# A three-stage kernel on one core: two stages in one block, one wait moved, one subtraction in halves, nine unread products

## The chip, the cores and the metric

The kernel runs on one core of a Trainium2 chip. The metric is the device time of one execution in microseconds (us). Five engines work side by side, each through its own list of instructions, and meet only at semaphores: TensorE (PE; its weight loads are PEld), VectorE (DVE), ScalarE (ACT), GpSimd (POOL) and SyncE (SP), which here only issues transfers. GpSimd also issues the indirect transfers (gather and scatter of rows).

## The reference, cut to what matters

```python
# stage 1, attention with a decaying state: 4 batches, 8 heads, 768 steps, head size 48
S = a * S + k[t] (outer) v[t]                  # a complex, its size bounded by 0.999
y[t] = q[t] @ S.real
# stage 2, on x = y as 3072 rows of 384
h = x @ w_in                                   # 384 -> 2048
x2 = (max(h, 0) + alpha * min(h, 0)) @ w_out   # 2048 -> 384
# stage 3, routed experts
do = x2 @ w_skip > 0                           # the other rows go out as they are
e = argmax(x2 @ w_gate)                        # one of 8 experts; gate = its softmax weight
out[do] = x2 + gate * (max(x2 @ w1[e], 0) @ w2[e])     # 384 -> 1024 -> 384
```

## The kernel before, in words

`build` makes the tensors that all stages share (the eight PSUM banks `mlp_ps`, `out_ps`, `att_ps`, the two halves `arena`, `rows`, `logits`) and calls `phase1` (stages 1 and 2) and then `phase2` (stage 3). Each phase opens a `Block` of its own: a block holds the instruction lists of the five engines, and at its end all engines meet before the next block starts. The SBUF tensors of phase 2 lie where those of phase 1 lay.

**Phase 1** walks over eight halves of 384 rows (`Half`). A half's attention runs beside the two products (`up`, `down`) of the half before. The work of each engine is written out by hand in `step`; the last half has no attention beside it and runs in the loop at the end of each engine's list. For each of 16 tiles `f` of the hidden width, TensorE makes `up(f)` (9 products, L646) into `mlp_ps`; ScalarE makes `bend_h` (L964); VectorE joins both in `join_g` (L1493); ScalarE and VectorE split the result into a high part and a remainder (`high_g` L972, `low_g` L1498); TensorE makes `down(f)` (9 products, L658) into `out_ps[0..2]`. `up(f)` waits for `join_g(f - 2)`, and the last half's list is `up(0)`, `up(1)`, `up(2)`, then `up(f)` and `down(f - 3)` in turn. On VectorE the wait `dve.wait_ge(state_moved, NC * HALVES * 64)` (L1967) stands ahead of the first `join_g` of that last half. `state_moved` counts SyncE's transfers of the attention state to `s_stack` (L382); the last four of them are issued behind the store of the second last half's rows. Nothing reads that last state. At the end ScalarE's `take_x2` (L985, L987) copies, for each of the three banks in turn, nine logits into `logits` and 384 values into `x2` (in `rows`), and SyncE stores `x2` to `out` and to `x2_rows` (L393, L394).

**Phase 2** first works out the routing: VectorE takes the largest logit and the membership (L2309 to L2324) with an index from GpSimd (L2469, L2471); TensorE counts ranks (L2172, L2173); VectorE works out each row's slot (L2337 to L2374) and then the entries of a table (`entries`, L2388), which TensorE sums with 24 products (L2181). Two copies out of the table give the rows to gather and to scatter (`gather_at` L2411, `scatter_at` L2412). GpSimd's `gather` (L2493) fetches 128 rows for a slot. For each slot TensorE turns the rows (L2188), makes the first layer (48 instructions, L2210), turns the next slot's rows, for which it waits until they have been gathered, and makes the second layer (24, L2224). The weights `w2` of an expert are split: ScalarE copies the high part (`split`, L2257), VectorE subtracts it (`split`, L2404, 128 x 3072). VectorE's `split(0)` stands behind the copies of the table, before `keep_x(1)`, which waits for the gathered rows. SyncE loads the weights of experts 1 and 2 at once and those of expert 3 when the first gather has landed (L2145, L2151). The slots of an expert stand in the code as `If` blocks and a loop, so their number is decided by branches.

Of the kernel before, what the change touches and what calls it, by code (L numbers as in the profile page):

```python
# [6 lines left out]
F32 = mybir.dt.float32  # L7
# [12 lines left out]
NC = 3  # L20
# [67 lines left out]
def val(count):  # L88

    return count.value() if isinstance(count, Count) else count  # L90
# [24 lines left out]
def build(nc, qk, v, a, mask_in, w_in, w_pack, alpha, w_skip, w_gate, w1, w2, out, x2_rows):  # L115
    with ExitStack() as ctx:
        def sem(name):
            return ctx.enter_context(nc.semaphore(name))

        def sb(name, shape, dt=F32):  # L120
            return ctx.enter_context(nc.sbuf_tensor(name, shape, dt))

        mlp_ps = [ctx.enter_context(nc.psum_tensor(f"mlp_ps{i}", [P, 512], F32)) for i in range(2)]
        out_ps = [ctx.enter_context(nc.psum_tensor(f"out_ps{i}", [P, 512], F32)) for i in range(3)]
        att_ps = [ctx.enter_context(nc.psum_tensor(f"att_ps{i}", [P, 512], F32)) for i in range(3)]

        ident = sb("ident", [P, P])
        logits = sb("logits", [P, NT, LANES])
        arena = [sb(f"arena{i}", [P, KT * FE]) for i in range(2)]
        rows = sb("rows", [P, NC * DL + DM])  # L130
        x2_stored = sem("x2_stored")
        first_loaded = [sem(f"first_loaded{i}") for i in range(2)]

        phase1(nc, qk, v, a, mask_in, w_in, w_pack, alpha, w_skip, w_gate, w1, w2, out, x2_rows,
               mlp_ps, out_ps, att_ps, ident, logits, arena, rows, x2_stored, first_loaded)
        phase2(nc, w1, w2, out, x2_rows, mlp_ps, out_ps, att_ps, ident, logits, arena, rows, x2_stored, first_loaded)


def phase1(nc, qk, v, a, mask_in, w_in, w_pack, alpha, w_skip, w_gate, w1, w2, out, x2_rows,
           mlp_ps, out_ps, att_ps, ident, logits, arena, rows, x2_stored, first_loaded):  # L140
    with ExitStack() as ctx:
        def sem(name):
            return ctx.enter_context(nc.semaphore(name))

        def sb(name, shape, dt=F32):
            return ctx.enter_context(nc.sbuf_tensor(name, shape, dt))

# [103 lines left out]
        g_lo = sem("g_lo")  # L251
        g_used = sem("g_used")
        x2_taken = sem("x2_taken")

        def att(h, name, c):

# [49 lines left out]
        def of_chunk(x, c):  # L306
            return x[..., c * DM:(c + 1) * DM]

        block = ctx.enter_context(nc.Block())


        @block.sync
# [538 lines left out]
        def _(act):  # L851
# [122 lines left out]
            def pair(n, f):  # L974
                if f < NF:
                    bend_h(n, f)
                if f >= 1:
                    high_g(n, f - 1)

            def take_x2(n):  # L980
                act.wait_ge(g_used, val(n.n * NF + (NF + 4)))
                act.wait_ge(x2_stored, val(n.n * 32 + 1))
                first = (n.n * NC).value()
                for i in range(NC):
                    act.activation(logits[:, bass.ds(first + i, 1), :].rearrange("p a l -> p (a l)"),  # L985
                                   out_ps[i][:, DM:DM + LANES], ACT.Copy)
                    act.activation(x2[:, i, 0:DM], out_ps[i][:, 0:DM], ACT.Copy).then_inc(x2_taken, 1)  # L987
# [304 lines left out]
            last_n = Half(0, HALVES - 1)  # L1292
            for f in range(NF + 1):
                pair(last_n, f)
            take_x2(last_n)


        @block.vector
        def _(dve):
# [664 lines left out]
                step(Half(0, n), True, True)  # L1964
            step(Half(0, HALVES - 1), True, False)
            last_n = Half(0, HALVES - 1)
            dve.wait_ge(state_moved, NC * HALVES * 64)  # L1967
            for f in range(NF + 1):
                pair(last_n, f)


        @block.gpsimd
        def _(pool):
# [6 lines left out]
            for bank in range(3):  # L1980
# [12 lines left out]
def phase2(nc, w1, w2, out, x2_rows, mlp_ps, out_ps, att_ps, ident, logits, arena, rows, x2_stored, first_loaded):  # L1993
    with ExitStack() as ctx:
        def sem(name):
            return ctx.enter_context(nc.semaphore(name))

        def sb(name, shape, dt=F32):
            return ctx.enter_context(nc.sbuf_tensor(name, shape, dt))
# [91 lines left out]
        w2_loaded = [first_loaded[1], *(sem(f"w2_loaded{p}") for p in range(1, BODY))]  # L2091
        w2_hi = sem("w2_hi")
        w2_lo = sem("w2_lo")
        expert_left = sem("expert_left")
        x_gathered = sem("x_gathered")
        x_turned = sem("x_turned")
# [7 lines left out]
        y_stored = sem("y_stored")  # L2104

        NP = NFE // 2
        block = ctx.enter_context(nc.Block())

        def expert(x, e):
            return x[e:e + 1]  # L2110
# [57 lines left out]
        def _(pe):  # L2168
# [5 lines left out]
            for t in range(NT):  # L2174
                if t % GROUP == 0:
# [3 lines left out]
                    else:  # L2179
# [2 lines left out]
                                 entries[t // GROUP][:, t % GROUP, :, :].rearrange("p a s -> p (a s)"),  # L2182
                                 start=(t == 0), stop=(t == NT - 1))
            last.then_inc(table_full, 1)

            def turn_x():
                for kk in range(KT):
# [49 lines left out]

        @block.scalar
        def _(act):
            act.wait_ge(diff_made, 1)  # L2240
            act.activation(expd[:, :, :], diff[:, :, :], ACT.Exp).then_inc(exp_made, 1)
            act.wait_ge(rows_known, 1)
            for t in range(NT - GROUP, NT):
                act.activation(far_off[:, t + GROUP - NT, :], lane[:, :], ACT.Abs, bias=row_of[:, t:t + 1], scale=-1.0).then_inc(distance, 1)
            act.wait_ge(distance, GROUP)
            act.activation(in_row[:, NT - GROUP:NT, :], far_off[:, :, :], ACT.Relu, bias=1.0, scale=-1.0).then_inc(late_rows_made, 1)

            def place_x(s):
                act.wait_ge(x_turned, val(s))
                act.activation(xT[:, :, :].rearrange("p k t -> p (k t)"), att_ps[0][:, 0:DM], ACT.Copy).then_inc(xT_made, 1)  # L2250

            def split(e):
                p = e % BODY
                if e >= BODY:
                    act.wait_ge(expert_left, e - BODY + 1)
                act.wait_ge(w2_loaded[p], e // BODY * 16 + 16)
                act.activation(w2_v[p][0][:, :, :], w2_raw[p][:, :, :], ACT.Copy).then_inc(w2_hi, 1)  # L2257

            count = act.alloc_register("act_slot")
            act.reg_mov(count, 1)  # L2260
            split(0)
            split(1)
            act.wait_ge(slots_known, 1)
            slots_here = slots_of_all(act)
            place_x(1)

            def expert_slots(e):
                n = slots_here[e]

                def split_next():  # L2270
                    if e + 2 < EXPERTS:
                        split(e + 2)

                def slot(is_first=False):
                    s = act.snap(count, min_val=1, max_val=NSLOT - 2)
                    act.wait_ge(b_done, val(s))
                    for g in range(NP):
                        act.wait_ge(h_full, val(s * 4 + (g - 3)))
                        act.activation(hT[:, 0, 2 * g:2 * g + 2, :].rearrange("p f t -> p (f t)"),  # L2279
                                       mlp_ps[g % 2][:, 0:2 * P], ACT.Relu).then_inc(h_hi, 1)  # L2280
                    place_x(s + 1)
                    act.reg_add(count, count, 1)
                    if is_first:
                        split_next()

                with act.If(n > 0):
                    slot(is_first=True)
                    act.nop()
                act.nop()
                if e + 2 < EXPERTS:  # L2290
                    with act.If(n < 1):
                        split_next()
                        act.nop()
# [8 lines left out]
        def _(dve):  # L2302
# [3 lines left out]
            def flat(x):  # L2306
                return x[:, :, :].rearrange("p e t -> p (e t)")

            dve.tensor_scalar(dropped[:, :], skip, 0.0, BIG, ALU.is_le, ALU.mult).then_inc(skips_placed, 1)  # L2309
            dve.tensor_reduce(out=top[:, :], in_=lg, op=ALU.max, axis=AX.X).then_inc(step, 1)  # L2310
            dve.wait_ge(step, 1)
# [89 lines left out]
            def split(e):  # L2401
                p = e % BODY
                dve.wait_ge(w2_hi, e + 1)
                dve.tensor_tensor(w2_v[p][1][:, :, :], w2_raw[p][:, :, :], w2_v[p][0][:, :, :].bitcast(F32), ALU.subtract).then_inc(w2_lo, 1)  # L2404

            dve.wait_ge(table_full, 1)
            dve.tensor_scalar(tab[:, :, 0], att_ps[1][:, 0:NSLOT], FAR, None, ALU.add).then_inc(tab_made, 1)
            dve.tensor_reduce(out=tab[:, :, 1].bitcast(F32), in_=att_ps[1][:, NCOL:3 * NCOL].rearrange("p (a s) -> p s a", a=2)[:, 0:NSLOT, :],
# [1 line left out]
            dve.wait_ge(tab_made, 2)  # L2410
            dve.tensor_copy(gather_at[:, :], tab[:, 0, 0:1]).then_inc(first_at, 1)  # L2411
            dve.tensor_copy(scatter_at[:, :], tab[:, NSLOT - 1, 0:1]).then_inc(first_at, 1)  # L2412
            split(0)
            dve.wait_ge(slots_known, 1)
            slots_here = slots_of_all(dve)
            keep_x(1)
            count = dve.alloc_register("dve_slot")
            dve.reg_mov(count, 1)
            dve.wait_ge(step, val(last_step))
# [43 lines left out]

        @block.gpsimd
        def _(pool):
            pool.sem_inc(b_done, 1)
            pool.sem_inc(y_made, 2)
            pool.sem_inc(h_lo, 4)
# [29 lines left out]
                                        bounds_check=TOKENS - 1, oob_is_err=False).then_inc(y_stored, 16)  # L2498

            pool.wait_ge(pads_made, 1)  # L2500
            pool.wait_ge(first_at, 2)
            gather()
            pool.memset(y[:, :], 0.0).then_inc(pads_made, 1)
            pool.wait_ge(slots_known, 1)
            slots_all = pool.value_load(slots_i[0:1, EXPERTS:EXPERTS + 1], min_val=0, max_val=NSLOT - 2)
# [93 lines left out]
```

## Time and profile before

| | |
|---|---|
| median of 3 timed runs | 857.11 us (855.49 to 857.2) |
| profiled execution, own time | 853.47 us |
| its span in the trace | 851.5 us |
| mean granted TensorE clock | 0.95 |
| busy: PE, PEld, DVE, ACT, POOL | 84%, 81%, 71%, 56%, 6% |

The span is what the trace covers; 1.97 us of the execution's time lie around it. Times in the rows are microseconds from the start of the span. A granted clock of 1.00 is 2.4 GHz and 0.50 is 1.2 GHz. Busy shares are means over stages with different limits, so they do not say what ends a stage; the rows do.

### The profile page before, as it was taken

To read this page: it belongs to the slowest core of one execution; us is meant where nothing else is said; L and a number is where in the kernel's file an instruction comes from. 1 tells how busy PE (TensorE), PEld (TensorE's weight loads), DVE (VectorE), ACT (ScalarE), POOL (GpSimd) and SP (SyncE) were. 2 spreads that over 40 slices of the span, in tenths; PEclk is the share of its full clock that TensorE was granted. 3 is DMA by queue.
4 is the path that set the end of the run, shared out by engine and by line. 5 is a ranking of instruction groups with operands and counts; after the bars stand their busy time and mean duration, and the time that the engine had idled before them with its cause. 6 is when DMAs were issued, how large, how long until landed. Compare 5 with 4: busy or idle time off the path is not lost. (4 is left out here: it accounts for less than half of the span.)

```text
span 851.5 us, 15352 instructions
## 1 busy us (share of the span) xinstructions
PE 718.7 (84%) x5454; PEld 693.5 (81%) x5454; DVE 607.5 (71%) x1250; ACT 478.3 (56%) x937; POOL 54.7 (6%) x56
## 2 busy tenths in 40 slices
PE   1213749999999999999999999999989639899895
PEld 1213749999999999999999999999889539799895
DVE  4986978997997997998899799654333454344442
ACT  8267369479559739937946964843423243233320
POOL 2000000000000000000000000000000122223222
PEclk9998769999999999999999999999989859899999
DMA  5465553345145325515515523442600376914200
GB/s 166 155 204 119 148 153 98 75 121 175 45 122 172 90 60 172 145 48 146 175 34 145 159 74 77 131 121 58 212 26 1 116 278 225 318 39 171 95 27 20
DMA packets 82429, 104.67 MB, mean 123 GB/s; under 512 B 15990, under 2 KB 68384, under 8 KB 82336
## 3 DMA queue, kind: packets, MB, share of 16 engines
q1 hardware_dynamic: 79648, 98.44, 38.9%
q0 software_dynamic: 1792, 3.76, 1.4%
q10 hardware_dynamic: 896, 1.25, 0.6%
q8 instruction: 56, 0.92, 0.5%
q14 instruction: 37, 0.30, 0.1%
HBM read 61.04 MB, written 12.19 MB: 86 GB/s over the span
## 5 line engine op out<-in xcount | busy, mean ns | idle before, releaser
L658 PE MATMUL out_ps<-w_out_hi,g_parts 128*128 128x394 f32 x768 | 219.8, 347 | 0.0
L646 PE MATMUL mlp_ps<-xT,w_in_hi 128*128 128x384 f32 x768 | 205.0, 349 | 14.8 <-DVE g L1493 13.9
L646 PEld LDWEIGHTS mlp_ps<-xT,w_in_hi 128*128 128x128 f32 x768 | 139.4, 192 | 21.7 <-DVE g L1493 19.7
L658 PEld LDWEIGHTS out_ps<-w_out_hi,g_parts 128*128 128x128 f32 x768 | 142.0, 188 | 2.6 <-issue 1.8
L646 PE MATMUL mlp_ps<-xT,w_in_lo 128*128 128x384 f32 x384 | 131.2, 342 | 0.0
L658 PE MATMUL out_ps<-w_out_lo,g_parts 128*128 128x394 f32 x384 | 131.0, 341 | 0.0
L1493 DVE SCALAR_TENSOR_TENSOR g<-mlp_ps,slope_side,bent 128x384 f32<-128x384 f32 x128 | 77.8, 613 | 67.7 <-ACT bent L964 59.4
L964 ACT ACTIVATE bent<-mlp_ps,bend_size 128x384 f32<-128x384 f32 x128 | 73.8, 577 | 92.0 <-PE mlp_ps L646 91.9
L972 ACT ACTIVATE g_parts<-g 128x384 fp32r<-128x384 f32 x128 | 66.2, 517 | 56.7 <-PE out_ps L658 49.7
L2279 ACT ACTIVATE hT<-mlp_ps 128x256 fp32r<-128x256 f32 x52 | 20.0, 384 | 100.2 <-PE mlp_ps L2210 100.2
L646 PEld LDWEIGHTS mlp_ps<-xT,w_in_lo 128*128 128x128 f32 x384 | 73.6, 192 | 0.0
L1498 DVE TENSOR_TENSOR g_parts<-g,g_parts 128x384 fp32r<-128x384 f32 x128 | 69.8, 551 | 3.9 <-ACT g_parts L972 3.6
L658 PEld LDWEIGHTS out_ps<-w_out_lo,g_parts 128*128 128x128 f32 x384 | 72.3, 188 | 0.0
L2432 DVE SCALAR_TENSOR_TENSOR hT<-mlp_ps,hT 128x256 fp32r<-128x256 f32 x52 | 22.1, 425 | 62.3 <-ACT hT L2279 62.3
L2210 PE MATMUL mlp_ps<-xT_e,w_sb 128*128 128x128 f32 x480 | 58.9, 285 | 8.7 <-issue 8.7
L2210 PEld LDWEIGHTS mlp_ps<-xT_e,w_sb 128*128 128x128 f32 x480 | 57.8, 200 | 10.2 <-issue 10.2
L737 PE MATMUL mlp_ps<-wgs,g 128*128 128x10 f32 x96 | 19.1, 329 | 52.4 <-ACT rows L1099 21.2
L737 PEld LDWEIGHTS mlp_ps<-wgs,g 128*128 128x128 f32 x96 | 18.5, 285 | 53.1 <-issue 32.1
L958 ACT ACTIVATE s_t<-s_in,f_pair 112x96 f32<-112x96 f32 x192 | 55.2, 362 | 6.9 <-DVE s_in L1475 6.9
L2224 PE MATMUL out_ps<-w_hi,hT 128*128 128x384 f32 x208 | 56.3, 342 | 0.0
L1448 DVE TENSOR_TENSOR qk_dec<-arena 128x768 f32<-128x768 f32 x48 | 45.1, 953 | 2.9 <-DMA kq<-qk_dec 1.5
L577 PE MATMUL att_ps<-kq 112*128 112x128 f32 x368 | 46.1, 279 | 0.1
(163 smaller groups left out, 1212.8 us busy)
## 6 DMA issues: line engine op xcount, KB each, us to landing
kq<-qk_dec SPq DMA_DIRECT2D x88, 144.0 KB, 3.0
arena<-in_a SPq DMA_DIRECT2D x24, 384.0 KB, 4.3
arena<-in_qk SPq DMA_DIRECT2D x24, 384.0 KB, 3.4
w_sb<-in_w SPq DMA_DIRECT2D x6, 1536.0 KB, 8.1
w_raw<-in_w SPq DMA_DIRECT2D x6, 1536.0 KB, 11.8
xT<-y_parts SPq DMA_DIRECT2D x48, 144.0 KB, 2.8
arena<-in_w SPq DMA_DIRECT2D x4, 1536.0 KB, 8.9
v_nat<-in_v SPq DMA_DIRECT2D x24, 192.0 KB, 3.9
```

The source lines that it names most:

```text
L577: last = pe.matmul(ps[:, n * CH:(n + 1) * CH], kq_of(h, c)[:, slot, 1, :], kq_of(h, c)[:, slot, 0, :], start=True, stop=True)
L646: last = pe.matmul(ps[:, 0:HT], w_in_v[s][:, kk, f * P:(f + 1) * P], xT[n.p][:, kk, m, :], start=(kk == 0 and j == 0), stop=(kk == KT - 1 ...
L658: last = pe.matmul(out_ps[i][:, 0:DL], g_parts[:, f % 4, s, i * P:(i + 1) * P], w_out_v[m][:, f, :], start=(f == 0 and j == 0), stop=(f == ...
L737: last = pe.matmul(mlp_ps[f % 2][:, 0:GATE_COLS], turned_stage[f % DEPTH][:, kk * P:(kk + 1) * P], wgs[:, kk, :], start=(kk == 0), stop=(k ...
L958: last = act.activation(s_t[:, r, :, pair_, :], s_in[:, :, pair_, :], ACT.Copy, scale=f_pair[:, h.p, pair_, c, r:r + 1])
L964: act.activation(bent[:, f % 2, :], mlp_ps[f % 2][:, 0:HT], ACT.Relu, scale=bend_size[:, f:f + 1]).then_inc(bent_made, 1)
L972: act.activation(g_parts[:, f % 4, 0, :], g[:, f % 3, :], ACT.Copy).then_inc(g_hi, 1)
L1448: dve.tensor_tensor(qk_dec[:, r, :, :, :], qk_raw[m][:, :, :, :], G, ALU.mult).then_inc(qk_made, 1)
L1493: dve.scalar_tensor_tensor(out=g[:, f % 3, :], in0=mlp_ps[f % 2][:, 0:HT], scalar=slope_side[:, f:f + 1], in1=bent[:, f % 2, :], op0=ALU.m ...
L1498: dve.tensor_tensor(g_parts[:, f % 4, 1, :], g[:, f % 3, :], g_parts[:, f % 4, 0, :].bitcast(F32), ALU.subtract).then_inc(g_lo, 1)
L2210: last = pe.matmul(mlp_ps[g % 2][:, (f % 2) * P:(f % 2 + 1) * P], w1_v[p][:, kk, f * P:(f + 1) * P], xT[:, kk, :], start=(kk == 0), stop=( ...
L2224: last = pe.matmul(out_ps[0][:, 0:DM], hT[:, a, f, :], w2_v[p][b][:, f, :], start=(f == 0 and j == 0), stop=(f == NFE - 1 and j == 2))
```

## The change

Phase 1 and phase 2 share one block that `build` opens. What the meeting of all engines ordered is now ordered by semaphores: ScalarE's last copies (`take_last`) take the three sets of logits first and count `logits_taken`, for which VectorE waits; GpSimd waits for the last `down`. VectorE's wait for the state stands behind the last half. ScalarE's `split(0)` stands behind the exponential. VectorE subtracts `w2[0]` in two halves, the first before the table is full, the second behind `keep_x(1)`. The first gather waits for `gather_at` alone. TensorE makes nine more products into `out_ps[1]`, which nobody reads, between the table and the first rows. The diff, cut to its core:

```diff
@@ build
+        block = ctx.enter_context(nc.Block())
+        g_used, logits_taken = phase1(..., sem, block)
+        phase2(..., sem, block, g_used, logits_taken)
@@ phase1, ScalarE
+            def take_last(n):
+                act.wait_ge(g_used, val(n.n * NF + (NF + 4)))
+                act.wait_ge(x2_stored, val(n.n * 32 + 1))
+                first = (n.n * NC).value()
+                for i in range(NC):
+                    act.activation(logits[:, bass.ds(first + i, 1), :].rearrange("p a l -> p (a l)"),
+                                   out_ps[i][:, DM:DM + LANES], ACT.Copy).then_inc(logits_taken, 1)
+                for i in range(NC):
+                    act.activation(x2[:, i, 0:DM], out_ps[i][:, 0:DM], ACT.Copy).then_inc(x2_taken, 1)
@@
             for f in range(NF + 1):
                 pair(last_n, f)
-            take_x2(last_n)
+            take_last(last_n)
@@ phase1, VectorE
             last_n = Half(0, HALVES - 1)
-            dve.wait_ge(state_moved, NC * HALVES * 64)
             for f in range(NF + 1):
                 pair(last_n, f)
+            dve.wait_ge(state_moved, NC * HALVES * 64)
@@ phase2
-        block = ctx.enter_context(nc.Block())
@@ phase2, TensorE
             last.then_inc(table_full, 1)
+            for _ in range(9):
+                pe.matmul(out_ps[1][:, 0:NT * EXPERTS], before_pp[:, :], members, start=True, stop=True)
@@ phase2, ScalarE
             act.activation(expd[:, :, :], diff[:, :, :], ACT.Exp).then_inc(exp_made, 1)
+            split(0)
             act.wait_ge(rows_known, 1)
...
             act.reg_mov(count, 1)
-            split(0)
             split(1)
@@ phase2, VectorE
+            dve.wait_ge(logits_taken, NC)
             dve.tensor_scalar(dropped[:, :], skip, 0.0, BIG, ALU.is_le, ALU.mult).then_inc(skips_placed, 1)
...
+            def split_half(part):
+                f = slice(part * NFE // 2, (part + 1) * NFE // 2)
+                return dve.tensor_tensor(w2_v[0][1][:, f, :], w2_raw[0][:, f, :], w2_v[0][0][:, f, :].bitcast(F32), ALU.subtract)
+
+            dve.wait_ge(w2_hi, 1)
+            split_half(0).then_inc(half_split, 1)
             dve.wait_ge(table_full, 1)
...
             dve.tensor_copy(scatter_at[:, :], tab[:, NSLOT - 1, 0:1]).then_inc(first_at, 1)
-            split(0)
             dve.wait_ge(slots_known, 1)
             slots_here = slots_of_all(dve)
             keep_x(1)
+            dve.wait_ge(half_split, 1)
+            split_half(1).then_inc(w2_lo, 1)
@@ phase2, GpSimd
+            pool.wait_ge(g_used, HALVES * NF + 4)
             pool.sem_inc(b_done, 1)
...
             pool.wait_ge(pads_made, 1)
+            pool.wait_ge(first_at, 1)
+            gather()
             pool.wait_ge(first_at, 2)
-            gather()
             pool.memset(y[:, :], 0.0).then_inc(pads_made, 1)
```

## Rows read from the trace of the kernel before

**Rows 1.** Busy time by stretch: us, each engine's busy time, PEclk, DMA share, GB/s.
```profile
621.00:626.70 5.70, 5.70 (x18) 5.70 (x19) 2.02 (x4) 1.41 (x3) 0.00 (x0) 0.51 0.00 0
```
**Rows 2.** Waits from 590 to 640: in total, times, longest, us.
```profile
DVE g L1493 <- DMA s_stack<-state: 7.4, 1, 7.4
PE mlp_ps L646 <- DVE g L1493: 5.1, 1, 5.1
```
**Rows 3.** Timeline at the last half's start: start us, us, engine, line, operation.
```profile
614.27 0.58 ACT L964 ACTIVATE bent<-mlp_ps,bend_size 128x384 f32<-128x384 f32 x1
...
615.46 0.34 PE L646 MATMUL mlp_ps<-xT,w_in_lo 128*128 128x384 f32 x1
...
620.24 1.14 DVE L1493 SCALAR_TENSOR_TENSOR g<-mlp_ps,slope_side,bent 128x384 f32<-128x384 f32 x2 [7.44 <-DMA s_stack<-state]
...
620.91 1.01 PE L646 MATMUL mlp_ps<-xT,w_in_hi 128*128 128x384 f32 x2 [5.11 <-DVE g L1493]
...
626.74 0.34 PE L658 MATMUL out_ps<-w_out_hi,g_parts 128*128 128x394 f32 x1
```
**Rows 4.** Timeline between the phases, with the first instructions of phase 2.
```profile
671.24 0.34 PE L658 MATMUL out_ps<-w_out_hi,g_parts 128*128 128x394 f32 x1
671.61 0.18 ACT L985 ACTIVATE logits<-out_ps 128x9 f32<-128x9 f32 x1 [4.63 <-PE out_ps L658]
...
674.43 0.70 SPq L2145 DMA_DIRECT2D w_sb<-in_w  x1
674.49 0.18 DVE L2309 TENSOR_SCALAR dropped<-logits 128x24 f32<-128x24 f32 x1 [6.91 <-PEq L141]
...
674.76 0.14 POOL L2469 IOTA e_index_i<- 128x8 int32 x1 [669.47 <-POOLq L141]
...
676.98 0.98 PE L2172 MATMUL mlp_ps<-member,before_pp 128*128 128x192 f32 x2 [5.40 <-DVE member L2324]
...
677.75 0.85 PE L2173 MATMUL mlp_ps<-member,ones_pp 128*128 128x192 f32 x2
```
**Rows 5.** Timeline from the table to the first slot.
```profile
688.21 3.66 PE L2181 MATMUL att_ps<-w_lo,w_hi 128*128 128x102 f32 x16 [0.46 <-DVE w_lo L2388]
688.54 1.01 DVE L2388 TENSOR_TENSOR w_lo<-w_raw,factor 128x816 fp32r<-128x816 f32 x1
...
692.27 0.15 DVE L2411 COPY gather_at<-tab 128x1 int32<-128x1 int32 x1
...
692.40 3.35 DVE L2404 TENSOR_TENSOR w_lo<-arena,w_hi 128x3072 fp32r<-128x3072 f32 x1
693.51 3.31 POOL L2493 DMA_INDIRECT rows<-x_rows,gather_at  x1 [15.72 <-issue]
...
698.96 0.90 PE L2188 MATMUL att_ps<-ident,rows 128*128 128x128 f32 x3 [7.09 <-DMA rows<-x_rows,gather_at]
...
700.53 7.80 PE L2210 MATMUL mlp_ps<-xT_e,arena 128*128 128x128 f32 x48 [0.67 <-ACT xT_e L2250]
```
**Rows 6.** Busy time by stretch while the weights load, columns as in rows 1.
```profile
693.00:694.50 1.50, 0.00 (x0) 0.00 (x0) 1.50 (x1) 0.00 (x0) 0.99 (x1) 0.50 0.78 270
694.50:696.00 1.50, 0.00 (x0) 0.00 (x0) 1.25 (x1) 0.00 (x0) 1.50 (x1) 0.50 0.02 5
```
**Rows 7.** Gathers, L2493: landing of all fourteen; then the second alone, its ns and landing.
```profile
DMA to landing us min/median/max: 2.5/5.4/6.6
...
L2493 POOL DMA_INDIRECT rows<-x_rows,gather_at x1: 1012/1012/1012, 700.7 to 700.7; - x1
DMA to landing us min/median/max: 6.6/6.6/6.6
```
**Rows 8.** Chain that ended last: two more slots' first layer, start us, us.
```profile
712.83 5.36 PE mlp_ps L2210 x48
...
736.52 8.54 PE mlp_ps L2210 x48
```
**Rows 9.** Waits of TensorE from 700 to 851.
```profile
PE mlp_ps L2210 <- issue: 10.1, 7, 4.0
```

More of the change, by code:

```diff
@@ L132, in build @@
         first_loaded = [sem(f"first_loaded{i}") for i in range(2)]
-        phase1(nc, qk, v, a, mask_in, w_in, w_pack, alpha, w_skip, w_gate, w1, w2, out, x2_rows,
-               mlp_ps, out_ps, att_ps, ident, logits, arena, rows, x2_stored, first_loaded)
-        phase2(nc, w1, w2, out, x2_rows, mlp_ps, out_ps, att_ps, ident, logits, arena, rows, x2_stored, first_loaded)
+        block = ctx.enter_context(nc.Block())
+        g_used, logits_taken = phase1(nc, qk, v, a, mask_in, w_in, w_pack, alpha, w_skip, w_gate, w1, w2, out, x2_rows,
+               mlp_ps, out_ps, att_ps, ident, logits, arena, rows, x2_stored, first_loaded, sem, block)
+        phase2(nc, w1, w2, out, x2_rows, mlp_ps, out_ps, att_ps, ident, logits, arena, rows, x2_stored, first_loaded,
+               sem, block, g_used, logits_taken)
 def phase1(nc, qk, v, a, mask_in, w_in, w_pack, alpha, w_skip, w_gate, w1, w2, out, x2_rows,
-           mlp_ps, out_ps, att_ps, ident, logits, arena, rows, x2_stored, first_loaded):
+           mlp_ps, out_ps, att_ps, ident, logits, arena, rows, x2_stored, first_loaded, sem, block):
     with ExitStack() as ctx:
-        def sem(name):
-            return ctx.enter_context(nc.semaphore(name))
         def sb(name, shape, dt=F32):
@@ L253, in phase1 @@
         x2_taken = sem("x2_taken")
+        logits_taken = sem("logits_taken")
         def att(h, name, c):
@@ L1990, in _, with phase2 @@
                                pattern=[[-1, P]], channel_multiplier=1).then_inc(consts, 1)
-def phase2(nc, w1, w2, out, x2_rows, mlp_ps, out_ps, att_ps, ident, logits, arena, rows, x2_stored, first_loaded):
+        return g_used, logits_taken
+def phase2(nc, w1, w2, out, x2_rows, mlp_ps, out_ps, att_ps, ident, logits, arena, rows, x2_stored, first_loaded,
+           kernel_sem, block, g_used, logits_taken):
     with ExitStack() as ctx:
         def sem(name):
-            return ctx.enter_context(nc.semaphore(name))
+            return kernel_sem(f"routed_{name}")
         def sb(name, shape, dt=F32):
@@ L2093, in phase2 @@
         w2_lo = sem("w2_lo")
+        half_split = sem("half_split")
         expert_left = sem("expert_left")
@@ L2106, in phase2 @@
         NP = NFE // 2
-        block = ctx.enter_context(nc.Block())
         def expert(x, e):
@@ L2239, in _, with split @@
         def _(act):
+            def split(e):
+                p = e % BODY
+                if e >= BODY:
+                    act.wait_ge(expert_left, e - BODY + 1)
+                act.wait_ge(w2_loaded[p], e // BODY * 16 + 16)
+                act.activation(w2_v[p][0][:, :, :], w2_raw[p][:, :, :], ACT.Copy).then_inc(w2_hi, 1)
             act.wait_ge(diff_made, 1)
             act.activation(expd[:, :, :], diff[:, :, :], ACT.Exp).then_inc(exp_made, 1)
+            split(0)
             act.wait_ge(rows_known, 1)
@@ L2250, in place_x @@
                 act.activation(xT[:, :, :].rearrange("p k t -> p (k t)"), att_ps[0][:, 0:DM], ACT.Copy).then_inc(xT_made, 1)
[L2252 to L2257, printed above, removed]
             count = act.alloc_register("act_slot")
             act.reg_mov(count, 1)
-            split(0)
             split(1)
```

## The prediction

> **What bounds the kernel now.** I read three views in this order: busy time and clock by stretch, the waits of each stage, and the timeline around the waits that TensorE itself suffers. Over the span TensorE is the busy engine, so a change pays where TensorE stands idle or runs at 1.2 GHz and something the change touches is the cause. There are two such places. At the start of the last half VectorE waits 7.4 us for the transfer of a state, and TensorE 5.1 us for VectorE [rows 2]; after it TensorE works at a granted clock of 0.51 for 5.7 us [rows 1]. Between the last `down` (ends 671.58) and the first slot's products (700.53) TensorE has little to do, while a serial chain runs: block end, routing on VectorE, table, gather [rows 4, 5]. From 700.53 on TensorE is the bound again, but for seven waits called "issue" of 10.1 us in all [rows 9].
>
> **The wait for the state moves behind the last half.** `up(0)` and `up(1)` are done when TensorE stops: its last product starts at 615.46, the next would start some 0.18 later, at 615.64; it starts at 620.91 [rows 3]. `up(2)` needs `join_g(0)`, which needs `bend_h(0)`, ready at 614.27 + 0.58 = 614.85 [rows 3]. A `join_g` is half of the pair that takes 1.14 us [rows 3], so it would be done by 615.5, ahead of 615.64. `bend_h(1)` follows `up(1)` at about 615.8, `join_g(1)` is done by 617.1, and `up(3)` asks for it only after nine products, at about 617.2. So the idle time goes whole: 620.91 - 615.64 = 5.27 us. The clock comes back as well. From 620.91 to 626.74 TensorE makes the 18 products of `up(2)` and `up(3)` in 5.83 us; at full clock one takes about 0.174 (`up(0)`, `up(1)` ran at that spacing ahead of 615.64), 3.13 in all, so 2.70 us. The moved wait is passed at once: the state had landed at 620.2, far ahead of the half's end. What is late next is TensorE itself. **8.0 us**; at least 5.3, where the clock would not have fallen anyway.
>
> **One block instead of two, logits first.** Before, VectorE's first routing instruction starts at 674.49, though the first logits were copied at 671.61 [rows 4]. Now it waits for three copies of 0.18 in a row: 672.15 at the latest, 672.0 if they overlap. The other order of the six copies moves no end: the rows of `x2` are as ready for the stores as before. SyncE goes from its second store straight to the weights, 0.4 us earlier than 674.43. GpSimd was the last to reach the index before (674.76); it is now let go when the last `down` ends, 671.6, has three increments and two small instructions to do (1.1 us in the trace of before), and so has the index at 672.7, ahead of the VectorE step that asks for it a microsecond after its start. Ranks, slots and table are a chain of VectorE and TensorE that moves with its start. **2.4 us** (2.3 to 2.5).
>
> **The first gather.** The table is full at 691.87 [rows 5], now 689.5. ScalarE's `split(0)` moves into its idle time before the rows are known and costs nothing; without it `split(1)` comes early enough as well. VectorE ends its entries at 689.55 [rows 5], now 687.15, and the first half of the subtraction (3.35 / 2 = 1.68) ends at 688.8, under the cover of TensorE's 3.66 us of table products [rows 5]. Then `gather_at` is ready at 692.42 - 2.4 = 690.0, and GpSimd starts 1.09 after it before, 0.06 less now that it does not wait for the second copy: 691.1. There the gather took 3.31 us on GpSimd while VectorE subtracted, and 1.01 for the second, which had no subtraction beside it [rows 5, 7]. The first landed 5.4 after its start, 2.1 after GpSimd was through. Quiet, it lands at 691.1 + 1.01 + 2.1 = 694.2. But the weight transfers run at full share until about 694.1 [rows 6], now 693.7 as they start only 0.4 earlier while the chain gained 2.4: the gather moves into their tail. The second gather, made wholly beside weights, took 6.6 [rows 7], which gives 697.7. I take 695.2: what is left of the 2.1 us when the weights end. Against 698.9 that is 3.7, of which 2.4 is counted: **1.3 us** (2.3 down to -1.2).
>
> The second gather shows what sharing cost here: 5.6 us after GpSimd was through, against 2.1 [rows 5, 7]. The Trainium skill (DMA: Bandwidth & Descriptors, Anatomy of one DMA) says that each transfer engine takes packets from its queues in turn; by that a small gather would about double its 2.1 us of transfer and land at 696.3 at worst; the term of 1.3 would then be 0.2 and the sum 11.6. The row speaks for more, and the measurement decides.
>
> **The nine products.** They start when the table is done, 689.5. The two rank products of the same shape take 0.77 from start to start and 1.62 together at a clock of 0.50 [rows 4]; the second has halves of about 0.33, so nine take 5.9 to 6.9 us and end at 695.4 to 696.4 if the clock stays low, earlier if it rises. That is as late as the gather, so they can cost up to 1.2. What they can bring: the first slot's 48 instructions took 7.80 us after a pause, 5.36 in a slot at full clock [rows 5, 8], and turning the rows 0.5 less: 2.9. TensorE worked 3.66 us on the table without the clock rising [rows 5, 6], so a rise is likely but not sure. Most of it is lost again: before its second layer TensorE waits for the second gather. Counted from the landing of the first, TensorE would ask for it at 1.1 + 5.36 = 6.5 at full clock (9.4 before: 708.33 - 698.91). GpSimd starts it 1.8 after the turning starts (700.73), 1.3 at full clock; 6.6 us beside the weights of expert 3, which the first gather's landing starts, make it 7.9. And the second half of the subtraction, moved there, runs from 0.5 to 2.2 and holds GpSimd up to 0.9 longer: 8.8. The gain is 9.4 less 7.9 to 8.8; I take **1.0 us** (2.9 down to -1.2). The first slot's second layer needs `w2_lo` only then, so the later remainder itself stops nobody.
>
> **Sum.** 8.0 + 2.4 + 1.3 + 1.0 = 12.7 us. The profiled execution's 853.47 (851.5 and 1.97 around it) becomes 840.8. The median of the runs lies 3.64 above that execution; nothing in the change bears on that difference, so the median goes from 857.11 to **844.4**.
>
> **Rivals.**
> 1. The gather meets the weights and the clock is not up in time: 8.0 + 2.4 - 1.2 + 0 = 9.2, 847.9. For it: the 6.6 of the second gather. Against: the weights end some 2 us after it starts. 20%.
> 2. The clock after the 5 us pause does not fall in most timed runs, so only the idle time goes: 12.7 - 2.7 = 10.0, 847.1. For it: a pause of 5.1 is short; against: it fell in the one seen. 14%.
> 3. The gather lands quiet and the second in time: 8.0 + 2.4 + 2.3 + 2.9 = 15.6, 841.5. Beyond it, with the 4.0 us wait [rows 9] and the half-clock slot behind it (8.54 - 5.36 [rows 8]) gone, up to 7.2 more: 834.3. 17%.
> 4. The change does not do what it says: the last half starts no earlier, something else comes with the state: 12.7 - 8.0 = 4.7, 852.4. Against: the `bent` it needs is there at 614.85. 4%.
> 5. Slower: TensorE waits for its own code. All positions after the table move by 36 instructions and the block's seams go; the seven "issue" waits stand at the slots' branches, 10.1 us in all, the longest 4.0 with a half-clock slot of 3.2 more behind it. The other six average 1.0; each that becomes like the longest costs 6.2. Two eat the gain (12.4), so from the third on the kernel is slower: 844.4 + 18.6 = 863.0. For it: the waits lie while weights load; against: as much may fall the other way. 5%, of which 2 are about no change. The Trainium skill (Runtime: NRT & Kernel Launch, Instruction fetch mechanics) says that a taken branch to code not yet on the chip waits for a transfer, which is this rival's mechanism; the trace's waits agree in place.
>
> **How the numbers follow.** The forecast has 40%. All unknown costs together reach from 834 to 853. I give 839.5 to 849.5: it holds the forecast, rivals 1 and 2 and the near part of 3; 4, 5 and the far part of 3 are left out. About 0.2% (1.7 us) is what a measurement can tell from no change. Faster by more: the forecast and rivals 1 to 4, 95%; within it 2%; slower 3%.
>
> **What would show it.** Right: no wait of VectorE for `s_stack` before the last half, TensorE without a pause there, the last `down` ending near 663.6; `dropped` 0.5 us after it; the first gather 1.0 long on GpSimd and landing 5 to 7 us after the table; a wait of TensorE for a gather at the end of the first slot. Wrong: TensorE still pausing for 5 us at the last half, a first slot of 7.8, or "issue" waits of more than 15 us in all.

## The result, and the profile after

The changed kernel took 842.97 us in the median of four runs (839.2 to 844.62), the kernel before 856.3 (854.88 to 857.2) beside it: a ratio of 0.984, 95% interval 0.9802 to 0.9877. In a second comparison, on another occasion, it was 0.9858 (0.9833 to 0.9883). That is 13.7 and 12.1 us off. The profiled execution has a span of 842.7, 8.8 less than the one of before.

The start of the last half, from the timeline of the changed kernel (columns as in rows 3), answers [rows 3]:
```profile
615.51 0.58 ACT L963 ACTIVATE bent<-mlp_ps,bend_size 128x384 f32<-128x384 f32 x1
...
616.13 0.62 DVE L1502 SCALAR_TENSOR_TENSOR g<-mlp_ps,slope_side,bent 128x384 f32<-128x384 f32 x1 [2.09 <-ACT bent L963]
...
616.88 0.54 PE L645 MATMUL mlp_ps<-xT,w_in_hi 128*128 128x384 f32 x2
```
VectorE now starts `join_g(0)` 0.04 us after `bent` is ready; before, it waited for the state there [rows 2]. TensorE's `up(2)` at 616.88 follows `up(1)` without a pause; before, 5.11 us lay between them [rows 3].

The chain that ended last, from the end of stage 2 to the second slot (start us, us, what):
```profile
658.45 6.43 PE out_ps L657 x36
664.90 0.33 ACT logits L984 x3
665.25 0.19 DVE dropped L2324
...
679.00 3.67 PE att_ps L2193 x16
...
684.23 5.74 DMA rows<-x_rows,gather_at
...
690.02 0.56 PE att_ps L2202 x3
...
691.23 7.20 PE mlp_ps L2224 x48
...
722.65 4.23 issue
```
Routing (from VectorE's `dropped` on) starts 0.37 after TensorE's last `down` (664.88), against 2.91 before [rows 4]. But the table is full at 682.67 and the rows land at 689.97, 7.30 later; before it was 7.04 [rows 5]. The first slot's first layer takes 7.20, before 7.80 [rows 5]. The longest "issue" wait of TensorE, 4 us, is still there [rows 9].

The timeline of the changed kernel around the nine products and the gather:
```profile
680.26 1.75 DVE L2423 TENSOR_TENSOR w_lo<-arena,w_hi 128x1536 fp32r<-128x1536 f32 x1
682.46 5.76 PE L2198 MATMUL out_ps<-member,before_pp 128*128 128x192 f32 x18
...
684.23 1.20 POOL L2516 DMA_INDIRECT rows<-x_rows,gather_at  x1 [15.96 <-DVE scatter_at L2433]
...
690.02 0.55 PE L2202 MATMUL att_ps<-ident,rows 128*128 128x128 f32 x3 [1.80 <-DMA rows<-x_rows,gather_at]
```
And busy time and clock by stretch there (columns as in rows 1):
```profile
687.00:688.50 1.50, 1.22 (x5) 0.92 (x4) 0.00 (x0) 0.00 (x0) 0.00 (x0) 0.75 0.64 220
688.50:690.00 1.50, 0.00 (x0) 0.00 (x0) 0.00 (x1) 0.00 (x0) 0.00 (x0) 1.00 0.04 10
690.00:691.50 1.50, 0.82 (x4) 0.59 (x5) 1.50 (x3) 0.49 (x1) 0.08 (x1) 0.89 0.39 33
691.50:693.00 1.50, 1.50 (x8) 1.50 (x9) 0.58 (x1) 0.00 (x0) 1.47 (x1) 0.50 0.79 276
```
The first half of the subtraction ends at 682.0, under the table's products, as meant. GpSimd is through in 1.20 instead of 3.31 [rows 5]. But the weights are still in transfer: the DMA share falls from full at about 687.8, and the rows land 2.2 later. The nine products raise the clock late in their run (0.75, then 1.00), then TensorE stands for 1.8 us, and when the first slot starts the clock is at 1.2 GHz again.

What the gather's packets met can be seen in the DMA queues: q0 carries GpSimd's gather (64 packets, 0.20 MB), q1 the weights, q8 instructions; the last figure is the share of the 16 transfer engines. From 687.1 to the landing:
```profile
q0 software_dynamic: 64, 0.20, 18.7%
q1 hardware_dynamic: 78, 0.10, 10.6%
q8 instruction: 1, 0.02, 2.4%
```
Before the change no weights were left there; from 697.0 to 699.0 in that kernel:
```profile
q0 software_dynamic: 64, 0.20, 36.3%
```
After GpSimd was through, the gather's first packet came 1.8 later (0.7 before the change), and first to last the packets took 2.3 (1.0 before).

### The profile page after: what moved, and what is told of

The parts are those of the page before. It is cut to its first block, busy times and chain, and to the rows that moved or that the text cites. A ratio compares the mean times of both kernels' runs of the same rounds, so it can differ in the third digit from the quotient of the medians.

```text
span 842.7 us, 15379 instructions
## 1 busy us (share of the span) xinstructions
PE 723.2 (86%) x5472; PEld 698.4 (83%) x5472; DVE 608.2 (72%) x1251; ACT 477.9 (57%) x937; POOL 53.1 (6%) x56
## 4 chain that ended last, share of the span: by engine, by line
PE 41%; DVE 24%; ACT 14%; issue 8%; SPq 6%; DMA 4%; POOL 0%; ACTq 0%; DVEq 0%; POOLq 0%
PE out_ps L657 9%; PE mlp_ps L2224 9%; PE mlp_ps L645 9%; PE out_ps L2238 6%; SPq L358 2%; ACT sq L925 2%; ACT s_t L957 2%; ACT L886 2%; DVE arena L1339 2%; DVE sq L1349 2%; DMA arena<-in_qk 2%; PE att_ps L576 2%; DVE g L1502 2%; DVE sq L1350 2%; SPq L373 2%
## 5 line engine op out<-in xcount | busy, mean ns | idle before, releaser
L645 PE MATMUL mlp_ps<-xT,w_in_hi 128*128 128x384 f32 x768 | 202.7, 345 | 10.6 <-DVE g L1502 9.6
L645 PEld LDWEIGHTS mlp_ps<-xT,w_in_hi 128*128 128x128 f32 x768 | 137.2, 190 | 17.6 <-DVE g L1502 15.3
L657 PEld LDWEIGHTS out_ps<-w_out_hi,g_parts 128*128 128x128 f32 x768 | 142.1, 188 | 2.6 <-issue 1.8
```

The costliest lines, as they stand in the source:

```text
L645: last = pe.matmul(ps[:, 0:HT], w_in_v[s][:, kk, f * P:(f + 1) * P], xT[n.p][:, kk, m, :], start=(kk == 0 and j == 0), stop=(kk == KT - 1 ...
L657: last = pe.matmul(out_ps[i][:, 0:DL], g_parts[:, f % 4, s, i * P:(i + 1) * P], w_out_v[m][:, f, :], start=(f == 0 and j == 0), stop=(f == ...
```

## The experiments

Each kernel was run against the kernel before on the same chip. For each profile the stages are measured from its own timeline, in us. The last half runs from its first product to the end of the last `down`; routing starts with `dropped`; the table is full when its last product ends; turning is TensorE's first work on the gathered rows; "rest" runs from the first slot's second layer to the end of the span:

| | last half | to routing | routing to table full | routing to turning | turning to 2nd layer | rest |
|---|---|---|---|---|---|---|
| before | 59.07 | 2.91 | 17.38 | 24.47 | 9.45 | 143.09 |
| changed, first profile | 51.11 | 0.38 | 17.41 | 24.77 | 8.49 | 144.19 |
| changed, second | 51.12 | 0.38 | 16.66 | 24.77 | 9.47 | 142.12 |
| e1: wait back | 58.46 | 0.38 | 17.41 | 24.75 | 8.74 | 143.19 |
| e4: moved wait alone | 51.15 | 2.89 | 17.37 | 24.44 | 9.55 | 143.05 |
| e7: moved wait, one block | 51.10 | 0.38 | 17.40 | 24.52 | 8.67 | 142.06 |
| e2: no products | 51.15 | 0.38 | 17.40 | 23.81 | 9.10 | 140.14 |
| e3: remainder whole | 51.12 | 0.38 | 17.39 | 24.82 | 8.54 | 139.08 |
| e5: expert 2 behind 1st gather | 51.15 | 0.39 | 16.66 | 22.09 | 8.54 | 142.75 |
| e6: fifteen | 51.15 | 0.38 | 16.67 | 26.03 | 8.54 | 135.97 |
| e9: fifteen, reads early | 51.10 | 0.38 | 17.25 | 24.79 | 8.63 | 138.25 |
| e10: experts 2, 3 behind 2nd | 51.12 | 0.38 | 16.69 | 22.23 | 6.91 | 145.73 |
| e11: e10, reads early, eight | 51.13 | 0.38 | 16.86 | 21.75 | 6.92 | 152.59 |
| e12: e11, no products | 51.10 | 0.38 | 16.86 | 21.75 | 9.27 | 148.93 |

The rows land 0.05 ahead of the turning, but for e5, e10 and e6, where TensorE comes 0.6, 0.7 and 1.5 after the landing. The table is full 0.7 earlier where the two rank products still ran at full clock (16.7 in the table). Without e10 to e12 the rest varies from 136 to 144, though the edits leave that code nearly untouched; so a small step can't be read from a whole span.

**e1_state_wait_back and e4_state_only: the moved wait, taken back and made alone.**

```diff
             last_n = Half(0, HALVES - 1)
+            dve.wait_ge(state_moved, NC * HALVES * 64)
             for f in range(NF + 1):
                 pair(last_n, f)
-            dve.wait_ge(state_moved, NC * HALVES * 64)
```

> The changed kernel with VectorE's wait for the state put back ahead of the last half; all else as changed. Theory 1 (the moved wait is the bulk of the gain, 8.1 us by the two profiles: 5.3 of pause and 2.7 of half clock): 842.97 + 8.1 = 851.1, and 848.3 where the clock doesn't fall in the pause; in the profile VectorE waits about 7.4 us for s_stack and TensorE pauses about 5.1. Rival (merging the blocks is the bulk, and the pause would have been filled anyway): at most 3 above the changed kernel, 846.

> The kernel before with only the wait for the state moved behind the last half. Theory 1: 856.3 - 8.1 = 848.2 (851.0 where the clock would not have fallen in the pause), with TensorE going on without a pause. Rival (the merged block is needed for the gain): 853 or more.

Taken back, the ratio to before is 0.9968 (0.9951 to 0.9984), 2.7 us. That is 9 to 11 us above the changed kernel, compared over two occasions, and 8.5 above e7, which ran beside it, where 8.1 was expected. Alone (the same lines the other way, in the kernel before) it is 0.9927 (0.9902 to 0.9951), 6.2 us, interval 4.2 to 8.4. TensorE's wait in the last half, with the wait put back:
```profile
PE mlp_ps L645 <- DVE g L1502: 5.1, 1, 5.1
```
The last half takes 51.10 to 51.15 in every profile without the wait ahead and 58.46 to 59.07 in the two with it. Theory 1 holds, and the block is not needed for the stage to shorten; the timed values for the move run from 6.2 (e4) to 11 us.

**e7_block_state: the moved wait and the one block, nothing else.** Against the changed kernel (ScalarE's `split(0)` goes back behind the rows too, which the cut leaves out):

```diff
-            for _ in range(9):
-                pe.matmul(out_ps[1][:, 0:NT * EXPERTS], before_pp[:, :], members, start=True, stop=True)
...
-            dve.wait_ge(w2_hi, 1)
-            split_half(0).then_inc(half_split, 1)
...
             dve.tensor_copy(scatter_at[:, :], tab[:, NSLOT - 1, 0:1]).then_inc(first_at, 1)
+            split(0)
...
             keep_x(1)
-            dve.wait_ge(half_split, 1)
-            split_half(1).then_inc(w2_lo, 1)
...
-            pool.wait_ge(first_at, 1)
-            gather()
             pool.wait_ge(first_at, 2)
+            gather()
```

> The changed kernel without the nine products and with the remainder whole at its old place, ScalarE's high part behind the rows again and the gather waiting for both copies: the moved wait and the one block alone. Theory 1 (8.1 and 2.5 add up): 856.3 - 10.6 = 845.7; VectorE's first routing instruction 0.4 after the last down against 2.9 before, and the gather landing about 7.0 after the table is full or later, since the weights now end later than the gather starts. Rival (the earlier routing is given back by the gather meeting the weight transfers): 847 to 848.

Ratio 0.9869 (0.9846 to 0.9891), 11.2 us (9.3 to 13.1) where the two steps' 10.6 were expected. The two add up within that interval. The rows land 24.47 after the routing's start, 24.42 before. What they waited for there was GpSimd: it is through only 22.36 after the routing's start, and between then and the landing (688.6 to 690.4) no weight packet is left:
```profile
q0 software_dynamic: 64, 0.20, 41.1%
```
The turning and the first slot took 8.67 together, 0.8 less than before, without any unread product.

**e2_no_nine: the changed kernel without the products.** The edit is the first two removed lines above.

> The changed kernel without the nine unread products. Theory 1 (they bring what the first slot shows, 1.0 us: its 48 instructions 7.20 instead of 7.80 and the turning 0.35 less): 844.0, first slot 7.8. Rival A (they bring nothing, since the clock fell again before the slot): 843.0, first slot 7.2 without them too. Rival B (they cost, by moving the code behind them): 842 or less, with the issue waits shorter than 10.2 in all.

Ratio 0.9865 (0.9842 to 0.9888), against 0.9858 (0.9833 to 0.9883) with them: nothing that can be told. Its first slot took 7.45, between the theory's 7.8 and rival A's 7.2. The rows landed 23.76 after the routing's start, 1.0 earlier than in the changed kernel and 0.7 earlier than in e7. From 685.4 to its landing:
```profile
q0 software_dynamic: 64, 0.20, 28.5%
q1 hardware_dynamic: 82, 0.10, 15.5%
```
The weights are there as in the changed kernel, but the packet of instructions (q8, 16 KB, 1.1 us long) is not; the gather's packets took 1.3 from first to last and not 2.3. All profiles with nine products or fifteen and this order of loads have that packet between 18.4 and 22.3 after the routing's start, and land at 24.5 to 24.8; e2 and e7 have none. That the products bring it, and that it delays the rows, fits these profiles, but is not shown: no run changes that alone.

**e8_changed: the changed kernel again, beside the next three.**

> The changed kernel itself, beside the next three and the kernel before on one chip. From the first comparison (ratio 0.984) and the kernel before at about 853 to 856 here: 839.5 to 842.5. Theory 1 (the nine products bring 1.0): 1.0 below the run without them (ratio 0.9865), so 0.985 or less; rival B (they cost): above 0.9865.

Ratio 0.9858 (0.9833 to 0.9883), not below e2's. The chain of this second profile:
```profile
685.39 6.48 DMA rows<-x_rows,gather_at
...
693.48 7.81 PE mlp_ps L2224 x48
```
Here the two rank products ran at full clock, and with them the table was full 0.75 earlier; the gather took 0.74 longer and landed the same 24.7 after the routing's start. TensorE's pause behind the nine products was 3.1, and the first slot took 7.81, as before the change.

**e3_whole: the remainder whole, with the products.** The edit is e7's without its first two lines.

> The changed kernel with the remainder whole at its old place, ScalarE's high part behind the rows and the gather waiting for both copies; the nine products and the block as changed. Theory (the first gather is held by the weight transfers, not by GpSimd's 3.3 us beside the subtraction): same as the changed kernel within 0.5; gather 3.3 us on GpSimd, landing 7.0 to 7.3 after the table. Rival (the halves bring what GpSimd saves, 2.1): 2 slower.

Ratio 0.984 (0.982 to 0.9861): not slower than the changed kernel. GpSimd took 3.32, and the rows landed 24.77 after the start. The time came out as the theory said, but not by its mechanism. From 685.8 to the landing:
```profile
q0 software_dynamic: 64, 0.20, 36.4%
```
The weights were in before the gather's first packet; here GpSimd's 3.3 us held it (through at 22.35), as in e7 and before the change. So the halves do remove what held the gather, and in the changed kernel the tail of the weights and the packet of instructions take its place; the two orders land within 0.1 of each other.

**e5_weights_late: expert 2's weights behind the first gather.**

```diff
-            for e in range(1, BODY - 1):
-                load_w1(e)
-                load_w2(e)
+            load_w1(1)
+            load_w2(1)
             sp.wait_ge(x_gathered, 16)
-            load_w1(BODY - 1)
-            load_w2(BODY - 1)
+            for e in range(2, BODY):
+                load_w1(e)
+                load_w2(e)
```

> The changed kernel with expert 2's two transfers (3 MB) issued behind the landing of the first gather, as those of expert 3 are. Theory (the weights in transfer hold the first gather): it lands 3.1 to 3.5 us after its start instead of 5.7, 4.7 to 5.1 after the table instead of 7.3, the nine products (5.8) then end last, TensorE's pause of 1.8 goes, the clock stays up and the first slot takes 5.4; it saves 1.5 there and up to 1.8 in the slot, less what the second gather then waits for, so 1 to 3 less than the changed kernel. Rival (the gather's own time is 5.7 whatever the weights do): the same as the changed kernel or slower, by the later weights.

Its first two gathers (ns on GpSimd, then landing, us):
```profile
L2516 POOL DMA_INDIRECT rows<-x_rows,gather_at x1: 1202/1202/1202, 684.4 to 684.4; - x1
DMA to landing us min/median/max: 3.3/3.3/3.3
...
L2516 POOL DMA_INDIRECT rows<-x_rows,gather_at x1: 1657/1657/1657, 689.7 to 689.7; - x1
DMA to landing us min/median/max: 6.7/6.7/6.7
```
The mechanism is shown: with no weights in transfer the same gather lands after 3.3 instead of 5.7 to 6.5. The gain is not: ratio 0.9862 (0.984 to 0.9885). The clock stayed up and the first slot took 5.6, but TensorE then waited for the second gather (6.7) and for the third (9.8), both beside weights:
```profile
PE att_ps L2202 <- DMA rows<-x_rows,gather_at: 2.7, 2, 1.4
```
The chain that ended last showed something else here: VectorE reads the eight slot counts one by one between the table and `keep_x(1)`, from 683.4 to 688.3, so the second gather could not start before 689.7.

**e6_fifteen: fifteen products instead of nine** (`range(9)` becomes `range(15)`).

> The changed kernel with fifteen unread products instead of nine. In the profile of the changed kernel the nine end 1.8 us before the gather lands and the clock, which had risen at about 687.5, falls again at 690.9. Theory (the pause makes it fall): six more at about 0.33 each end 2.0 later, TensorE has no pause, the clock stays up, the first slot takes 5.4 us instead of 7.2; then the second gather (6.6 after its start) ends last, 2.5 or less saved of it: 0.5 to 1.5 less than the changed kernel. Rival (TensorE's work doesn't decide it): same.

Ratio 0.9828 (0.9804 to 0.9851), 1.0 to 2.6 us under the two comparisons of the changed kernel, with intervals that overlap. Not for the reason I gave:
```profile
681.83 7.25 PE L2198 MATMUL out_ps<-member,before_pp 128*128 128x192 f32 x30
...
691.39 0.54 PE L2202 MATMUL att_ps<-ident,rows 128*128 128x128 f32 x3 [2.31 <-issue]
...
692.60 7.25 PE L2224 MATMUL mlp_ps<-xT_e,arena 128*128 128x128 f32 x48 [0.67 <-ACT xT_e L2272]
```
The rows had landed at 689.90, but TensorE still had its own reads of the eight counts to do, which stand behind the products: a pause of 2.3, the clock fell, the slot took 7.25. What is lower in this profile is the rest, 135.97, with 5.3 us of "issue" waits in it; no part of that is shown to come from the edit.

**e9_reads_fifteen: fifteen, with TensorE's reads of the counts ahead of the table.**

```diff
             pe.matmul(mlp_ps[1][:, 0:NT * EXPERTS], ones_pp[:, :], members, start=True, stop=True).then_inc(ranked, 1)
+            pe.wait_ge(slots_known, 1)
+            slots_here = slots_of_all(pe)
...
-            for _ in range(9):
+            for _ in range(15):
...
-            pe.wait_ge(slots_known, 1)
-            slots_here = slots_of_all(pe)
```

> Fifteen unread products, and TensorE's reads of the eight slot counts ahead of the table instead of behind the products. With fifteen and the reads behind them TensorE still paused, 2.3 us, for the reads, and the first slot took 7.25. Theory (it is TensorE's pause that lets the clock fall): the turning starts with the landing or within 0.3 of the products' end, the first slot takes 5.4, the second gather (6.3 to 6.7) ends it, so 8.5 from the turning to the second layer, as before; about 1 us less than with the reads behind (0.9828), of which the reads are 1.5 and the clock nothing. Rival (the clock falls whatever TensorE does there): first slot 7.2 again.

Ratio 0.9811 (0.9778 to 0.9844), the lowest of all; it beats the kernel before, and whether it beats the changed kernel is not settled (the intervals overlap). The turning started with the landing, but the clock had risen early in the products (0.69, then 1.00), so they ended 1.2 us ahead of it; the clock fell once more and the slot took 7.25. My 5.4 was wrong: the pause was shortened, not closed.

**e10_weights_second, e11_all_three, e12_no_products: experts 2 and 3 behind the second gather.** The edit is e5's with `sp.wait_ge(x_gathered, 32)`; e11 adds e9's reads with eight products, e12 the reads with none.

> The changed kernel with expert 2's and expert 3's weights issued behind the landing of the second gather. Behind the first alone, the first landed in 3.3 but the second took 6.7 and the third 9.8 us. Theory (weights in transfer are what makes a gather slow): first and second land 3 to 3.5 after their starts, the first 4.9 and the turning 5.4 after the table instead of 7.3, the second layer of the first slot 7 after the turning instead of 8.5: 3.4 us less than the changed kernel, less what the third gather then loses (6.7 to 9.8 beside the weights against about 8 that it has): net 1.5 to 3.4 less. Rival (the cost only moves to the third gather): same as the changed kernel within 1.

> The changed kernel with TensorE's reads ahead of the table, expert 2's and 3's weights behind the second gather, and eight products. Theory: the eight end about 5.0 after the table, with the landing, no pause, the clock up, first slot 5.4, second layer 7.0 after the turning: 0.5 below the run with the weights alone, 2 to 4 below the changed kernel. Rival (the third gather takes it back): same as the changed kernel.

> The same as the last with no unread products: what they bring once the gathers don't hide it. Theory: the first slot at half clock, 7.8 instead of 5.4 and the turning 0.5 less: 2.5 to 2.9 slower than with the eight. Rival (they bring nothing even then): the same.

Ratios 0.9912 (0.9878 to 0.9946), 0.9903 (0.9871 to 0.9934) and 0.9931 (0.9902 to 0.9959). The front did what the theory said: the first gather took 3.3, the second 3.6, and turning to second layer 6.9 in e10 and e11. The rest took it back (145.7 to 152.6, against 142.1 and 144.2): by the ratios the three lie 4 to 8 us above the changed kernel, over different occasions, e11 with intervals that overlap, and above e9, timed beside them, with intervals that do not. In the chain of e10 it was not at the third gather (9.9 us to its landing) but here:
```profile
694.54 10.47 DMA w_raw<-in_w
...
707.70 0.37 ACT hT L2293
708.10 0.44 DVE hT L2454
708.58 4.76 PE mlp_ps L2224 x24
```
ScalarE's `split(2)` stands at the end of the first slot in its list, two experts ahead, and waits 8.2 us for the weights, whose transfer takes 10.5; the second slot's `hT` is queued behind it, and TensorE waited 5.4 for that. e11 and e12 differ by the eight products alone. TensorE's timeline in e11:
```profile
680.90 4.84 PE L2200 MATMUL out_ps<-member,before_pp 128*128 128x192 f32 x16
685.99 0.55 PE L2204 MATMUL att_ps<-ident,rows 128*128 128x128 f32 x3 [0.25 <-DMA rows<-x_rows,gather_at]
687.20 5.62 PE L2224 MATMUL mlp_ps<-xT_e,arena 128*128 128x128 f32 x48 [0.67 <-ACT xT_e L2272]
```
With 0.25 us between the products and the turning the clock stays up; e12's same stretch takes 9.27 instead of 6.92, 2.35 more. Timed side by side the medians differ by 2.2 us (847.36 and 845.16), with intervals that overlap: in this stretch the products bring what was expected of them, and only when they reach the landing.

## Why the prediction was right, point by point

The time, 842.97 for 844.4, and the gain, 12.1 to 13.7 for 12.7, lie where they were put. The four terms did not fare alike: the first two (10.4) came as forecast, the other two (2.3) did not, so that the sum came out this near is in part luck.

- **The wait for the state, 8.0: right.** 59.07 became 51.11, 7.96 less, the pause and the half-clock stretch both gone. The part that hangs on the clock (2.7) can't be told in the timed runs: e4 saved 6.2, interval 4.2 to 8.4, which holds both 8.0 and 5.3.
- **One block, logits first, 2.4: right.** 2.91 became 0.38: 2.53. GpSimd's index was not late.
- **The first gather, 1.3: wrong.** Seen from the routing's start, the rows landed at 24.4 before and 24.7 after; the step's 1.3 is a loss of 0.3. The failed step is "what is left of the 2.1 us when the weights end". In the prediction's times, counted from its routing start at 672.1, I had the weights at full share until 21.6 and the rows landing 1.5 later, at 23.1. They were at full share until about 22.5, and the rows landed 2.2 later. The halves took away GpSimd's 2.1 us, as meant, and the gather then ran into the tail of the weights: it was through on GpSimd at 20.2, first packet at 21.9, last at 24.3. Without the nine products it landed at 23.8 (e2), 0.7 earlier than with neither step (e7, 24.5); with weights held back it landed at 21.5 to 21.7. The Trainium skill's rule (DMA: Bandwidth & Descriptors, Queues, rings and completion order, the section behind the one that the prediction names), that the engines take packets from their queues in turn, gave 24.2, and the loaded row 25.6; of the three values 24.2 is the nearest to the 24.7 measured. No run here shows the rule by itself: the packets took 2.3 us from first to last there, but 1.3 in e2, also beside weights, and 1.0 alone.
- **The nine products, 1.0: not shown.** The stretch from the turning to the second layer was 0.96 shorter in one profile and no shorter in the other; without any product it was 0.8 shorter in e7 and 0.35 in e2. So the 0.96 is luck. The first slot started at 1.2 GHz, or the clock fell to it within 0.8 us, in every profile but e5, e10 and e11, and what it took hangs on when the clock rose inside it: 2.9 us after its start in e7 (7.01), 3.3 in the changed kernel (7.20), 3.9 in e2 (7.45), 4.6 before and in e8 (7.80, 7.81), 4.8 in e4 (7.89). What I left out is the pause: I had the products end as late as the gather lands, but the clock rose while they ran, they ended 1.8 and 3.0 before the landing, and the clock fell again. And the rows may land 1.0 later for them (e2). The second gather did not hold the first slot in the changed kernel, which the prediction had named as a sign. It did in e5, where the clock stayed up: it landed 8.8 after the first, the end of the 7.9 to 8.8 that I had worked out, though there VectorE's reads had held its start.
- **The signs.** Three of the signs of being right are there (no wait for the state, `dropped` at 0.4, GpSimd 1.2 long for 1.0). The landing came 7.3 after the table, where 5 to 7 was forecast. Of the signs of being wrong one is there, in the second profile: a first slot of 7.81.
- **Waits called "issue" (rival 5).** 10.2 against 10.1 us. The same TensorE code gave 6.6, 8.2, 8.3, 9.6 and 10.2 in five profiles (e3, e8, e5, e1 and the changed kernel), so they vary from one execution to the next by more than the small terms of the sum; the shift of position was not needed to explain any of it. That they are waits for code is argued: in the changed kernel a packet of the instruction queues lies in, or ends within 1 us ahead of, each of the four longest (1.0 to 4.2 us), and none beside the other two (0.6 and 0.7).

The stages of the two profiles give 8.0 + 2.5 - 0.3 + 1.0 (or 0) = 10.2 to 11.2; the timed ratio says 12.1 to 13.7, with intervals 2 to 3 us to either side. From the routing's start to the second layer the changed kernel took 33.3 and 34.2, e7 33.2: steps three and four together bring nothing there. Where the other 1 to 3 us come from is open; the rest of the kernel varies by as much between profiles of one code.

## What to carry to other kernels

A wait that only guards data nobody reads is free only where its engine has nothing behind it: put it where its engine's list ends, and look in the waits for an engine whose neighbours pause with it. Before making a late transfer earlier, look at what else is on the transfer engines at that moment; moved into the neighbours' tail, it can lose there what its earlier start gained. When two orders end alike, look whether the same thing held both: here it was GpSimd in one and the weights in the other. Work that only keeps a clock up has to reach up to the work it serves: nine products that end 1.8 us early brought nothing that could be told, eight that end 0.25 us before it brought 2.35 us of that stretch. And before a stage's gain is put down to an edit, look at a kernel without the edit: e7 had most of the 0.96.

## What the runs showed of the hardware that was not expected

- A gather of 128 rows took 3.3 us to land with the transfer engines free, 4.8 (e2) to 6.5 in the tail of weight transfers, and up to 9.9 beside two experts' weights.
- The same gather kept GpSimd 1.2 us alone and 3.3 us beside VectorE's subtraction of 3.35 us; then it landed 5.4 to 5.7 after its start with no weights in transfer (before, e4, e7, e3).
- A packet of 16,384 bytes in an instruction queue took 1.1 us on the transfer engines in the middle of the gather (the changed kernel, e1, e8); e2, without it, landed 1.0 earlier. That the one makes the other is not shown.
- TensorE paused between the unread products and the turning for 1.2 us in e9 and 1.8 to 3.1 in the changed kernel, e1, e3, e6 and e8, followed by 0.7 around the turning; in all six the clock went to half, from 2.2 us ahead of the first slot (e8) to 0.8 us into it (e9). With pauses of 0.07 (e10), 0.25 (e11) and 0.5 (e5) it stayed at 2.4 GHz through the first slot. The last three have weights held back as well; no run separates the two.
- Reading eight counts into registers took VectorE 5 us (e5), and TensorE's reads, put behind fifteen products, kept it 1.5 us past the landing (e6).
